# The opening of an attention and two-layer kernel in a new order: the first tile of tokens works on its own keys alone

## The reference

```python
# 1: attention, 8 heads of 64, window of 128 keys
scores = q @ k.T / 8 - slope[h] * |i - j|     # where 0 <= i - j < 128, else -1e9
attn = exp(scores - rowmax); attn /= rowsum + 1e-9
x = attn @ v                                  # (2304, 512)
# 2: "SoLU" layer, 512 -> 1024 -> 512
h = x @ w_in
solu = h * softmax(h)
x = layernorm(solu) * g_ln @ w_out
# 3: gated layer, 512 -> 1536 -> 512
y = (silu(x @ w_gate) * (x @ w_val)) @ w_out
```

## Time and profile before

| | us |
|---|---|
| median of 3 runs | 723.54 |
| lowest, highest | 722.55, 723.68 |
| the profiled execution, its own time | 723.24 |
| its span (first to last instruction) | 721.5 |

### The profile page before, as it was taken

One profiled execution on the slowest core, in us unless ns is written; L12 is line 12 of the kernel. 1 busy time (PEld: TensorE's weight loads), 2 busy tenths in 40 slices (PEclk: granted clock), 3 DMA queues, 4 the chain that ended last, 5 costly groups with the idle time before them and its releaser, 6 DMA issues.

```text
span 721.5 us, 13261 instructions
## 1 busy us (share of the span) xinstructions
PE 712.7 (99%) x4748; PEld 683.2 (95%) x4748; DVE 481.3 (67%) x851; ACT 414.9 (58%) x847; POOL 387.8 (54%) x398
## 2 busy tenths in 40 slices
PE   8999999999999999999999999999999999999998
PEld 7878999999999999999999999999999999999998
DVE  4888777777777777756885655555546699754650
ACT  5897777777777776664634434343433388255340
POOL 3685444544544455884938957759576937300000
PEclk9999999999999999999999999999999999999999
DMA  8932453333343323034234342324336665895822
GB/s 336 317 106 75 153 184 118 130 116 119 128 143 119 116 74 117 15 117 146 78 107 136 117 142 100 131 88 154 106 106 241 236 229 202 279 377 186 275 87 88
DMA packets 49340, 109.92 MB, mean 152 GB/s; under 512 B 3984, under 2 KB 30352, under 8 KB 49296
## 3 DMA queue, kind: packets, MB, share of 16 engines
q1 hardware_dynamic: 49296, 109.33, 43.9%
HBM read 75.11 MB, written 34.21 MB: 152 GB/s over the span
## 4 chain that ended last, share of the span: by engine, by line
PE 95%; DVE 1%; DMA 1%; ACT 1%; issue 1%; POOL 0%; SPq 0%; POOLq 0%
PE banks L619 35%; PE banks L778 18%; PE banks L605 15%; PE banks L578 14%; PE banks L564 4%; PE banks L550 2%; PE banks L591 2%; PE banks L541 2%; PE banks L542 2%; PE banks L528 1%; DMA early<-in_early 1%; POOL wout_lo L1470 0%; ACT wo_hi L796 0%; DVE xs_lo L1183 0%; DVE p_own L1123 0%
## 5 line engine op out<-in xcount | busy, mean ns | idle before, releaser
L619 PE MATMUL banks<-xs_hi,w_hi 128*128 128x384 f32 x504 | 168.7, 335 | 0.4 <-ACT g_sum L796 0.4
L619 PE MATMUL banks<-xs_hi,w_lo 128*128 128x384 f32 x504 | 168.4, 334 | 0.0
L619 PE MATMUL banks<-xs_lo,w_hi 128*128 128x384 f32 x504 | 168.4, 334 | 0.0
L619 PEld LDWEIGHTS banks<-xs_hi,w_hi 128*128 128x128 f32 x504 | 94.6, 188 | 1.3 <-ACT g_sum L796 0.7
L619 PEld LDWEIGHTS banks<-xs_lo,w_hi 128*128 128x128 f32 x504 | 94.6, 188 | 0.0
L619 PEld LDWEIGHTS banks<-xs_hi,w_lo 128*128 128x128 f32 x504 | 94.6, 188 | 0.0
L605 PE MATMUL banks<-lnt_hi,wout_hi 128*128 (+1 forms) x288 | 85.5, 297 | 0.6 <-POOL wout_lo L1470 0.6
L778 PE MATMUL banks<-lot_hi,wo_lo 128*128 128x384 f32 x252 | 84.2, 334 | 0.0
L778 PE MATMUL banks<-lot_hi,wo_hi 128*128 128x384 f32 x252 | 84.2, 334 | 0.0
L778 PE MATMUL banks<-lot_lo,wo_hi 128*128 128x384 f32 x252 | 84.2, 334 | 0.0
L796 ACT ACTIVATE g_sum<-banks 128x384 f32<-128x384 f32 x84 | 41.2, 490 | 70.0 <-PE banks L619 54.6
(11 more groups left out here) (100 smaller groups left out, 1720.3 us busy)
## 6 DMA issues: line engine op xcount, KB each, us to landing
lot_raw<-unit_scratch SPq DMA_DIRECT2D x63, 384.0 KB, 4.8
qk_raw<-in_qk SPq DMA_DIRECT2D x28, 768.0 KB, 4.3
unit_scratch<-st_sums SPq DMA_DIRECT2D x18, 576.0 KB, 4.4
unit_scratch<-st_even SPq DMA_DIRECT2D x18, 384.0 KB, 2.5
unit_scratch<-st_odd SPq DMA_DIRECT2D x18, 384.0 KB, 3.2
w_raw<-in_wb SPq DMA_DIRECT2D x12, 512.0 KB, 4.7
v<-in_v SPq DMA_DIRECT2D x18, 256.0 KB, 2.6
x_scratch<-x_out SPq DMA_DIRECT2D x18, 256.0 KB, 2.6
```

Of the source, the lines that this page charges most:

```text
L619: last = mm(ps[n % 2], w_of[l][:, k * P:(k + 1) * P], x_of[r][:, k * HALF:(k + 1) * HALF], start=start and k == 0 and i == 0, stop=k == 1 ...
```

## The change

What it does:

1. Tile 0 makes scores of its own 128 keys only (`first_scores`), POOL fills `fold` with the masked value before any data is there, `copy_prev` of tile 0 and the zeroed v tile are gone, `unfold` makes only `p_own`, and `attend(0, 0)` has half its products.
2. The mask `own_q` comes also in slot 8 of group 0's first operands (`E_MASK`), so `select_own` of tile 0 waits for these and not for `const`. Group 0's operands come in two transfers, heads 0 and 1 (256 KB), then heads 2 and 3 and the mask (320 KB); group 1's have 512 KB.
3. Tile 0's probabilities are scaled by DVE (`scale_first_probs`), no longer by POOL.
4. All five openings are in a new order. Piece 0's low part goes from POOL to DVE, piece 1's from DVE to POOL, piece 3's from POOL to DVE. `keep_warm` goes from 6, 5 and 5 to 4, 5 and 3.

The diff, cut to its core:

```diff
-E_Q, E_K, E_NONE, E_SLOTS = (0, 13), (4, 9), 8, 17
+E_Q = ((0, 1, 4, 5), (13, 14, 15, 16))
+E_K = ((2, 3, 6, 7), (9, 10, 11, 12))
+E_MASK, E_SLOTS = 8, 17
...
+        first_own_q = early[0][:, E_MASK:E_MASK + 1, :].bitcast(I32)
...
-            return (win_lo_pool, win_lo_dve, win_lo_dve, win_lo_pool)[n], 1 + n // 2
+            return (win_lo_dve, win_lo_pool, win_lo_dve, win_lo_dve)[n], (1, 1, 2, 3)[n]
...
@@ sync @@
-                load_early(0, 0)
-                load_early(0, 1)
+                load_first(0, slice(0, 4), first_in)
+                load_first(0, slice(4, E_MASK + 1), early_in[0][0])
+                load_first(1, slice(0, E_MASK), early_in[0][1])
+                load_piece(0)
+                load_early(1, 0)
                 sp.dma_start(const[:, :], const_d).then_inc(const_in, 16)
-                load_early(1, 0)
                 load_early(1, 1)
-                load_piece(0)
                 load_piece(1)
+                load_piece(2)
                 load_v(0, 0)
-                load_piece(2)
                 load_piece(3)
                 load_early(2, 0)
...
@@ tensor @@
+            def first_scores(g, heads=range(4)):
+                pe.wait_ge(first_in if g == 0 and heads[0] == 0 else early_in[0][g], 16)
+                into = ps_h if g else scores
+                for i in heads:
+                    last = mm(into[:, i // 2, i % 2 * 256:i % 2 * 256 + P], early[g][:, E_Q[0][i], :],
+                              early[g][:, E_K[0][i], :], start=True, stop=True)
+                if heads[-1] == 3:
+                    last.then_inc(scores_ready, 1)
...
+                sides = ((odd, p_own),) if is_at(t, 0) else ((odd, p_own), (1 - odd, p_prev))
...
-                keep_warm(6)
-                early_scores(0, 0)
-                early_scores(0, 1)
+                keep_warm(4)
+                first_scores(0, range(0, 2))
+                first_scores(0, range(2, 4))
+                first_scores(1)
+                keep_warm(5)
                 early_scores(1, 0)
-                early_scores(1, 1)
                 pe.wait_ge(const_in, 16)
                 transpose_probs(0, 0)
-                keep_warm(5)
+                early_scores(1, 1)
                 transpose_probs(0, 1)
-                keep_warm(5)
-                pe.wait_ge(zeroed, 1)
+                keep_warm(3)
                 attend(0, 0)
                 early_scores(2, 0)
                 pe.wait_ge(selected, 4)
-                hidden(0, 0, 0)
+                hidden(0, 0, 0, range(0, 3))
                 transpose_probs(1, 0)
+                hidden(0, 0, 0, range(3, CM))
...
+                early_scores(3, 1)
+                transpose_probs(2, 1)
                 hidden(1, 1, 1)
-                transpose_probs(2, 1)
-                early_scores(3, 1)
                 attend(2, 0)
                 transpose_ln(0, 0, 0)
+                hidden(2, 0, 0, range(0, 1))
+                transpose_ln(0, 1, 0)
+                hidden(2, 0, 0, range(1, CM))
...
@@ scalar @@
-                copy_prev(0, 0, 0)
-                copy_prev(0, 1, 0)
                 exp_scores(0, 0)
+                piece(0)
                 exp_scores(0, 1)
-                piece(0)
...
@@ vector @@
+            def scale_first_probs(g):
+                dve.wait_ge(inv_ready, g + 1)
+                inv = pinv[:, g, :].rearrange("p (h a) -> p h a", a=1).to_broadcast([P, 4, P])
+                nc.vector.tensor_tensor(fold[:, g, :, :], fold[:, g, :, :], inv, ALU.mult).then_inc(probs_ready, 1)
...
-                dve.wait_ge(const_in, 16)
+                dve.wait_ge(early_in[0][0], 16)
                 select_own(0, 0, 0)
                 find_max(0, 0)
                 select_own(0, 1, 0)
                 find_max(0, 1)
                 invert_sums(0, 0)
+                scale_first_probs(0)
+                piece(0)
+                dve.wait_ge(const_in, 16)
+                unfold(0, 0)
                 invert_sums(0, 1)
-                unfold(0, 0)
+                scale_first_probs(1)
...
@@ gpsimd @@
-                nc.gpsimd.memset(v[:, 1, :], 0.0).then_inc(zeroed, 1)
+                nc.gpsimd.memset(fold[:, :, :, :], HD ** 0.5 * MASKED).then_inc(prev_copied, 2)
+                pool.wait_ge(prev_copied, 2)
                 pool.wait_ge(const_in, 16)
-                pool.wait_ge(zeroed, 1)
-                put_positions(0)
-                scale_probs(0, 0)
-                scale_probs(0, 1)
-                piece(0)
-                piece(3)
+                piece(1)
                 scale_probs(1, 0)
                 scale_probs(1, 1)
+                piece(4)
...
```

142 lines of the change are left out of this document (76 added, 66 removed).

## The result

The changed kernel takes 726.49 us (median of 22 executions, 723.22 to 729.58); the kernel before, run beside it on the same chip, 723.96 (22 executions, 722.55 to 726.73). The ratio is 1.0033, 95% interval [1.0019, 1.0047]: slower, 5.5 us above the forecast of 721.0.

A forecast was written before the change was run, and what follows sets the result against it. The transfer queue and the ACT, DVE and POOL chain awaiting it pace the first 20.85 us; PE bounds from 57.07 on. Gains of 1.6 and 0.7, 2.3 us off 723.24, give 720.9, stated as 721.0; range 719.8 to 722.7.

The forecast's parts named there:

- three signs of being wrong: Tile 2's load outside 16.3 to 18.5; filler behind 8 us still 0.24 us; hidden to layer1_out not under 36.2.
- The cover of tile 4's operands: Tile 4's raw operands, moved back on SP, ready by 50 us and wanted at 51, covered by at least one microsecond.
- The second term: From hidden to first layer1_out: stalls fall from 3.0 to 2.3, gaining 0.7 us; bounds nothing to 1.5.
- The price of `const`: In the opening's transfer queue: const costs 2.2 us, not its size's 0.95, and the same in sixth place.
- the cut of group 0's load: In the opening: tile 0's group 0 in two loads, landing at 3.4 and 4.2 us, with no added cost counted.
- rival D: Opening's queue: const costs only its size at its new place, one microsecond better, 719.9 us; chance 0.10.
- The first term: Opening up to hidden(0, 0): starts at 19.1 to 19.3 instead of 20.85, set by tile 2's load; gain 1.6 us.
- Rival C: Loads don't come as added up, or stalls of tiles 1 to 3 grow: 0.5 us net, 722.7; chance 0.12.
- Rival B: Opening: PE's low clock level lasts until 11 to 14 us, hidden slips 0.5 to 1.4, 721.4 to 722.4; chance 0.12.
- The rule named in the prediction: PE's clock: low by default, released only by sustained activity, brought back by a quiet stretch; weighed for the opening's gaps.
- Rival E: Opening: low clock level still there when hidden should begin, which starts 3.9 us late, 726.4; chance 0.05.
- the mask's 2.9 us: Tile 0: select_own no longer waits for const, so DVE is 2.9 us earlier; not the gain, since the transpose awaits const.

The follow-up runs named there:

- e7: The changed kernel with the loads of tile 4's raw operands and piece 7 and the split of tile 3's last keys placed as before: 724.05 us.
- e10: e7 with tile 0's group 0 operands in one load of 576 KB instead of two: 722.10 us.
- e11: e10 with longer filler runs in the opening, keep_warm 6 and 9 in place of 4 and 5: 721.44 us.
- e5: e4 with tile 0's mask also moved into its first operands, one load for each group: 723.13 us.
- e13: e11 with the late load of tile 4's raw operands put back in: 723.80 us.
- e6: The changed kernel with PE's and DVE's order around tile 1's hidden layer as in the kernel before: 728.74 us.
- e4: The kernel before with only tile 0's scores cut to its own keys, the mask still from const: 723.00 us.
- e1: The changed kernel with the split of tile 4's operands moved later on ACT and POOL: 727.18 us.

## Why the prediction was wrong, step by step

The forecast was 721.0 and the measured median is 726.49. Taking the faults out one after the other gives 724.05 (`e7`, 2.4 us), 722.10 (`e10`, 2.0 us) and 721.44 (`e11`, 0.7 us, not told from nothing). The sum is 5.05 of the 5.5. Of the three signs of being wrong that the prediction named, two came: the filler behind 8 us still took 0.23 us a product, and the stretch from `hidden` to `layer1_out` was 40.55 and not shorter than 36.2. Tile 2's load, the third, landed at 18.3, inside its bounds.

- **The cover of tile 4's operands, "ready by 50, wanted at 51".** This step failed, and it cost most. It asked when PE wants them. ACT wants them first, at 38.8 (37.75 + 1.06), because `split_qk(4, 0, 0)` stands in its queue ahead of what feeds tile 2's `hidden`. What is queued behind that wait was never listed. Before, the same load was issued at 25.93 and landed 6.1 us later, and ACT didn't wait for it. The change puts it behind tile 3's operands, v and piece 7 on SP, and behind the split of tile 3's keys on ACT and POOL; it is issued at 34.60 and lands at 40.4. The stretch to `layer1_out` became 40.55 us where 35.5 were forecast.
- **The second term, 0.7 us.** Wrong also without that fault. In `e7`, `e10` and `e11` the stretch is 36.3 us, before 36.2. The largest stall is 1.58 where 1.7 to 1.8 was forecast, so the size of that one is right, though the parts named for it (39.1 + 1.10 + 1.19 + 0.68) give 42.1 and not the 43.2 that it was taken from. The four stalls of before add up to 2.9, not 3.0. By the profile's waits the stretch has 2.4 us of them before, 2.4 in `e7` and 1.9 in `e11`; the 0.4 that `e11` is better there is lost again in the pace of the products, for which no run shows a cause. The bound "nothing" was the value.
- **The price of `const`, 2.2 us wherever it stands, and the cut of group 0's load, taken as free.** The number was right and its owner wrong. In its new place `const` lands 1.0 us behind tile 1's operands (2.61 + 7.7 = 10.3, then 11.3), which is what its size takes: rival D's premise. The extra microsecond belongs to the third place in the queue; in `e10` piece 0 pays it. The change cut group 0's load in two and so put group 1, for which PE waits, into that place, and the cut itself costs the queue about one more. Group 1 landed 2.3 us late, piece 0 and tile 1's group 0 as much, and the rest, `const` having cost less than taken, by about one. The first term came out as a loss of 0.4 where 1.6 of gain was forecast, and with one load it was 1.9 (`e10`).
- **Rival C** had this cause, a smaller first load and loads that don't come as added up. Its price was too small: 0.5 us net over all, 722.7, where `e7`, with the cut and without the late load, has 724.05.
- **Rival B, the low level until 11 to 14 us.** It happened, until about 12.5, and its price of 0.5 to 1.4 was right (1.06). The 0.12 was too low: "PE has no gap at all from 5.5 on" rested on group 1's landing at 5.5, so the two faults weren't independent. In `e10` the low level is there too, until about 9 us, and `hidden(0, 0)` begins at 18.98, behind 1.12 us of waiting for tile 2's load: it costs only where no load is waited for.
- **The clock behind a stall.** No rival had it. The rule named in the prediction, that of the Trainium skill ("TensorE: Matmul & The Clock Gate", "What's actually happening"), that a quiet stretch brings the low clock back, was weighed for the opening only. The trace agrees with it at 45 us: 2.90 us of waiting, then 0.50 for six microseconds. Behind the 1.58 of `e7`, close to the stall of 1.7 to 1.8 that was forecast, the clock stayed up.
- **Rival E** forecast 726.4, near the measured time, but the low level was gone nine microseconds before `hidden`. The agreement is chance.
- **Right:** the first scores at 3.5, the gain of the opening once its faults are out, `layer1_out` shifting the end one for one (664.33 before, 664.41 in `e11`), and the mask's 2.9 us being no gain by themselves.

Open: why the third transfer is late in all of these profiles, and what in the cut slows the queue by another microsecond. The third landing differed by 1.1 us between two profiles with the same queue, so a single profile doesn't tell.

## What to carry to other kernels

When a load or a copy is moved back, look for the first engine that touches it and for what that engine has queued behind, not for the last consumer. A price read between two landings belongs to a place and a time in the queue until it has been seen to move with the transfer. A PE stall of two microseconds or more may bring slow products behind it, as most of those here did, and these belong in its price. Where it can't be removed, filler products are a cheap test of whether the clock has a part in the loss.

## What the runs showed of the hardware

- The clock: PE gaps of 2.19, 2.90, 3.53 and 4.05 us were followed by the low level (granted clock 0.66 over 8 to 12 us in `e5`, 0.50 from 48 to 54 in the change, 0.50 from 46 to 48 in `e13`, 0.54 from 49 to 51 in `e6`). Those of 1.08 (`e4`) and 1.58 (`e7`) weren't, and that of 2.21 in `e1` wasn't either, so near two microseconds it went both ways.
- What the slow stretch costs beside the gap differs: about 3.0 us against 1.3 in the change's profile, 0.8 against 1.95 in `e13`'s. Filling the gap brought back 2.4 us of the median.
- The time goes with the mean clock among executions of one kernel: 722.31 at 1.000 and 725.08 at 0.995 in `e13`. `e11`, with no gap over 1.58 us, has 721.42 to 721.54 in its five executions; `e7`, with none over 1.72, still has 722.70 to 725.45.
- The low level at the start doesn't show in the granted clock's column of the change (1.00 from 8 to 12 us), only in the lengths: 0.23 us a product of 128 columns against 0.13.
- The first transfers: the one in third place landed between 6.6 and 8.3 us in 14 profiles, with 576 to 1152 KB ahead of it. With the first load cut in two, about 2500 KB had landed at 11.1 to 11.8 us in six of seven profiles, against 9.4 to 10.4 in the seven without the cut.
